# Four of the low parts of expert 1 made between the gathers of slots 7 and 8 instead of before all gathers

## The reference, cut to what matters

```python
x = attn_out.transpose(0, 2, 1, 3).reshape(B * S, H * D)
logits = xn @ en.T / tau                  # xn, en: rows of unit length
expert_idx = np.argmax(logits, axis=1)
gate_w = probs[np.arange(N), expert_idx]
for e in range(E):
    mask = expert_idx == e
    h = np.maximum(x[mask] @ w1[e], 0.0)
    out[mask] = gate_w[mask, None] * (h @ w2[e])
```

## Time and profile before

| what | value |
|---|---|
| median of 3 runs | 1118.97 us (1118.86 to 1122.63) |
| the profiled execution | 1119.63 us, of it the span 1118.0 us |
| mean granted TensorE clock | 0.977 |
| busy in the span | PE 94%, PEld 78%, DVE 57%, POOL 52%, ACT 45% |
| chain that ended last | PE 57%, POOL 6%, DMA 5% |

### The profile page before, as it was taken

The page is one execution under the profiler, slowest core; times in us unless marked ns, Lnnn a source line. Parts: engine busy times, 40 slices in busy tenths (PEclk is TensorE's granted clock), DMA queues, the critical chain, the costliest instruction groups (busy, mean ns, idle before and its releaser), DMA issues.

```text
span 1118.0 us, 21568 instructions
## 1 busy us (share of the span) xinstructions
PE 1050.3 (94%) x6536; PEld 873.2 (78%) x6536; DVE 631.7 (57%) x1477; ACT 508.5 (45%) x1035; POOL 579.8 (52%) x680
## 2 busy tenths in 40 slices
PE   7999999999993998999999995799999999999998
PEld 5777777777762887788888884698989999999997
DVE  6878878787856222121222212567767667676664
ACT  4666767666644222222222211355544545555543
POOL 3333333333334787877670602885656556565554
PEclk9999999999995999999999997899999999999999
DMA  4642414322345789989971814510101001010000
GB/s 118 177 116 80 112 55 118 89 78 80 99 156 158 245 255 266 300 282 308 301 244 54 268 49 130 180 29 2 57 1 57 1 6 52 0 56 0 29 1 29
DMA packets 102628, 129.62 MB, mean 116 GB/s; under 512 B 39520, under 2 KB 56928, under 8 KB 102048
## 3 DMA queue, kind: packets, MB, share of 16 engines
q1 hardware_dynamic: 78096, 68.38, 20.1%
q0 software_dynamic: 18880, 53.22, 15.5%
q10 hardware_dynamic: 5584, 7.16, 1.8%
HBM read 112.74 MB, written 15.99 MB: 115 GB/s over the span
## 4 chain that ended last, share of the span: by engine, by line
PE 57%; POOL 6%; DMA 5%; issue 2%; DVE 1%; ACT 1%; POOLq 0%; SPq 0%; DVEq 0%; ACTq 0%
PE ps L1032 17%; PE ps L1034 17%; PE ps L1033 17%; DMA stage<-w 3%; POOL wl L551 3%; PE ps L1058 1%; POOL woutl L551 1%; POOL wh L562 1%; PE ps L972 1%; PE ps L1028 1%; DMA wouth<-w_out 1%; PE ps L1107 1%; PE ps L982 1%; POOL xs_far L588 0%; ACT junk L773 0%
## 5 line engine op out<-in xcount | busy, mean ns | idle before, releaser
L551 POOL TENSOR_TENSOR wl<-stage,wh 128x512 fp32r<-128x512 f32 x128 | 161.9, 1290 | 60.6 <-DMA stage<-w 52.9
L663 POOL TENSOR_TENSOR mg<-mw,mr 128x384 f32<-128x384 f32 x96 | 118.6, 1235 | 75.4 <-DVE mr L1463 75.3
L711 ACT ACTIVATE ex<-sc,rmin 128x576 f32<-128x576 f32 x144 | 111.5, 775 | 94.7 <-DVE sc L1234 94.3
L1032 PE MATMUL ps<-yth,winh 128*128 128x384 f32 x384 | 132.6, 345 | 7.9 <-DVE mw L1451 7.9
L667 POOL TENSOR_TENSOR gl<-mg,gh 128x384 fp32r<-128x384 f32 x96 | 97.5, 1016 | 76.8 <-ACT gh L842 76.8
L1234 DVE TENSOR_SCALAR_CACHE_REDUCE sc<-ps,nscale 128x576 f32<-128x576 f32 x144 | 117.1, 814 | 28.6 <-PE ps L886 23.8
L1034 PE MATMUL ps<-yth,winl 128*128 128x384 f32 x384 | 130.6, 340 | 0.0
L1033 PE MATMUL ps<-ytl,winh 128*128 128x384 f32 x384 | 130.3, 339 | 0.0
L517 POOL TENSOR_SCALAR thr<-rmin,taup 128x1 f32<-128x1 f32 x144 | 66.2, 460 | 101.0 <-DVE sc L1234 100.0
L1034 PE MATMUL ps<-wouth,gl 128*128 128x512 f32 x288 | 114.2, 396 | 0.0
L1033 PE MATMUL ps<-woutl,gh 128*128 128x512 f32 x288 | 114.0, 396 | 0.0
(11 more groups left out here) (201 smaller groups left out, 2430.6 us busy)
## 6 DMA issues: line engine op xcount, KB each, us to landing
wh<-w POOLq DMA_DIRECT2D x32, 1024.0 KB, 9.1
stage<-w SPq DMA_DIRECT2D x128, 256.0 KB, 4.6
y_sorted<-yo ACTq DMA_DIRECT2D x25, 256.0 KB, 4.4
q_t<-qT SPq DMA_DIRECT2D x16, 288.0 KB, 2.8
k_t<-kT SPq DMA_DIRECT2D x16, 288.0 KB, 3.2
vb<-v SPq DMA_DIRECT2D x16, 288.0 KB, 3.4
out<-os SPq DMA_DIRECT2D x18, 256.0 KB, 3.1
stage<-w_in SPq DMA_DIRECT2D x16, 256.0 KB, 3.0
```

The costliest lines, as they stand in the source:

```text
L551: g.tensor_tensor(dst, raw, src.bitcast(F32), ALU.subtract).then_inc(w_split, 1)
L663: g.tensor_tensor(mg[:, f % 2, :], mw[:, f % 2, :], mr[:, f % 2, :], ALU.mult).then_inc(g_done, 1)
L711: act.activation(ex[:, i % 2, t * S:(t + 1) * S], sc[:, i % 2, t * S:(t + 1) * S], ACT.Exp, bias=rmin[:, i % 2, t:t + 1], scale=-1.0).then ...
L1032: pe.matmul(out_, lhs_h, rhs_h, start=start, stop=False)
```

## The change

Low quarter 1 of expert 1, four TENSOR_TENSOR on POOL with their waits, is moved from before the gathers to between gather 7 and gather 8 (2 * FIRST is 8).

```diff
         for i in range(QUARTERS):
             load_quarter(1, 1, i)
-        for i in range(2):
-            low_quarter(1, 1, 1, i)
+        low_quarter(1, 1, 1, 0)
...
         g.wait_ge(placed, 1)
-        for s in range(NEAR):
+        for s in range(2 * FIRST):
+            gather(s)
+        low_quarter(1, 1, 1, 1)
+        for s in range(2 * FIRST, NEAR):
             gather(s)
         g.wait_ge(gates_kept, 1)
```

## The result

| kernel | median | ratio to before, 95% interval |
|---|---|---|
| before | 1120.48 us (15 runs) | 1 |
| changed | 1125.01 us (15 runs, 1120.94 to 1127.34) | 1.0037 (1.0024 to 1.0049) |
| changed, measured again (e8) | 1122.59 us (12 runs) | 1.0026 (1.0013 to 1.0039) |
| changed, a third time (e11), on another chip | 1123.10 us (12 runs) | 1.0003 (0.9987 to 1.0018) |

A forecast was written before the change was run, and what follows sets the result against it. POOL's arrival at expert 2's loads was taken to bound the kernel: 2.5 us gained on DVE, 5.1 added on POOL, so 1118.97 + 2.6 = 1121.6 us, 0.23% slower; range 1118.2 to 1125.2.

The forecast's parts named there:

- The bound: Between the gathers and 475.6 us POOL sets the time; its arrival at expert 2's loads, 378.44, shifts all that follows.
- The gain on DVE: Before the gathers, three DVE operations freed from POOL's low parts bring the first gather 2.5 us earlier (2.35 to 2.66).
- the upper bound of 0.61: L1327 undisturbed on DVE takes at most 0.61 us, its end behind POOL's boundary; 0.45 was taken.
- the strict rule: A blocked DVE operation has its whole duration still ahead: L1327 needs 0.61 us, gain 2.35, sum 2.75; not adopted.
- The cost on POOL: Between gathers 7 and 8, four low parts add 5.1 us to POOL's way to expert 2's loads, nothing on DVE.
- the forecast sum: POOL reaches the loads of expert 2 at 378.44 - 2.5 + 5.1 = 381.04, 2.6 us later (2.4 to 2.8).
- it moves as a block: All in POOL's stretch from expert 2's loads to 475.5 us, issued by POOL or on its signals, shifts together by 2.6.
- slot 9 at 478.2, after a wait of about 1.5: PE starts slot 9 at 478.2 us in the profile after, released by POOL after waiting about 1.5 us.
- rival D: The longer gap puts slot 9's wait in a low clock or doubles the low time: at most 2.8 us, 1124.4; 0.05.
- Behind it nothing has changed its place relative to PE: After slot 9 starts, the rest of the kernel follows PE as before, so the end moves by the same 2.6 us.
- a longer wait at slot 7 costs no more: PE's slot 7 wait grows from 3.92 to about 9.0 us, with no larger low-clock loss than the 2.83 us before.

The follow-up runs named there:

- e8: The changed kernel again, no edit, on the chip of a later run; 1122.59 us, ratio 1.0026 to before.
- e11: The changed kernel a third time, no edit, on another chip; 1123.10 us, ratio 1.0003 to before.
- e1: The changed kernel with quarter 1's four low parts ahead of gather 0, behind the wait for placed, not between gathers 7 and 8; 1122.28 us, ratio 1.0020 to before.
- e4: The kernel before with quarter 1's low parts made on DVE in its idle time behind inv_i, none on POOL; 1119.30 us, ratio 0.9984 to before.
- e2: The kernel before, quarter 1 in its old place, plus four further subtractions on POOL between gathers 7 and 8; 1124.57 us, ratio 1.0030 to before.
- e3: The changed kernel with 30 transposes of the identity on PE ahead of m1 of slot 9; 1123.36 us, ratio 1.0022 to before.
- e5: As e4, with quarter 2 of expert 1 made on DVE too, behind its work for slot 0; 1113.49 us, ratio 0.9945 to before.
- e9: As e5, with quarter 3 of expert 1 made on DVE too, in its work for slot 1; 1114.39 us, ratio 0.9923 to before.
- e12: The kernel before, unchanged, measured against itself with a second profile; 1122.53 us, ratio 0.9990.

## Why the prediction was right, and where it was off

**The bound.** Right. e1 moved the start of slot 0 by 3.9 us at no cost. Counted from the first load of expert 1, POOL's arrival at the loads of expert 2 moved by -1.7 us in e4, +2.2 in e1, +2.6 in the changed kernel and in e8, and +3.9 in e2; the times moved, in the order of these kernels, by -1.8, +2.2, +4.1 and +2.9, and +3.4. All of these are on chips whose profiles show no holds; the +0.3 of e11 does not fit the row. "POOL's clock starts at 378.44, and whatever shifts that moment shifts all that follows" is what the runs show, to within about 1.5 us.

**The gain on DVE.** Forecast 2.5 us (2.35 to 2.66), measured 2.18 in the pair of profiles: 0.28 + 0.95 + 0.95. The term that was off is L1327. Alone it takes 0.77 us, above the upper bound of 0.61. The bound was read as the time from POOL's boundary to the operation's end. The two neighbours ended 0.15 and 0.17 us behind theirs while taking 0.31 alone, so some 0.15 us of an operation is already behind it when it is let go; 0.61 + 0.15 gives 0.76. The prediction had both numbers in hand and used them only against the strict rule. That the gain hangs on when the stage chunks land was missed altogether: it was 1.51 in e2. In the second profile of the kernel before the disturbed durations were 0.72, 0.31, 1.39 and 1.25, or 1.98 us above the undisturbed ones. The first gather still came at 349.48 against the forecast 349.6, since the attention ended 0.3 us earlier in that execution: that much of the agreement is luck.

The Trainium skill, "SBUF — State Buffer", section "Who interferes with whom", named the right pairs: of the operations beside POOL, those with two SBUF inputs were long, and the reduction at L1322, which lay wholly beside POOL, took 0.30 us before and after. That the later one is blocked for the whole of the other agrees with the ends: 0.15, 0.17 and 0.61 us behind POOL's boundaries. What the prediction called the strict reading, in which a blocked operation has all of its own duration still ahead of it, does not agree: those durations are 0.31, 0.31 and 0.77 us.

**The cost on POOL.** Forecast 5.1, measured 4.9: the next gather started 5.21 us behind gather 7's end, of which 0.30 stood there before. No DVE operation was slowed in the new place. The arrival at the loads, counted from the first load of expert 1, moved from 56.56 us (378.44 - 321.88) to 59.17 (380.73 - 321.56), by 2.6: the forecast sum. Gain and cost were each forecast 0.2 us too large, and cancel: from the first load to the first gather it is 2.3 us less, from there to the loads 4.9 more.

**The step that failed** is "it moves as a block", with "slot 9 at 478.2, after a wait of about 1.5". Slot 9 came 98.5 us behind POOL's arrival in place of 97.2, through other stage waits. POOL's waits from the loads to 480 us after:

```profile
POOL wl L551 <- DMA stage<-w: 22.4, 9, 5.8
```

The prediction had 20.8. PE had also reached slot 9 sooner, since slot 7 to slot 8 took 14.11 us against 15.08. The two add up to a wait of 4.15 us, and the clock fell: 1.6 us more. The event is that of rival D, given 0.05 and priced at up to 2.8. Its mechanism, that the longer gap at slot 7 brings it about, is not what the runs show: e4 with 5.00 us at slot 7 and e1 with 2.88 had waits at slot 9 of 3.56 and 4.39 us, and the clock fell in both. What they show is that the prediction took as fixed what scatters between executions: the stage waits (slot 9 stands 97.2 us behind the loads in one profile, 98.1 to 99.8 in seven others), the loss after slot 7 (2.8 us in one profile, 1.5 to 2.8 in the others), and the part behind the slots. "Behind it nothing has changed its place relative to PE" holds to about 2 us only, as the last slot shows. The prediction rightly said that a longer wait at slot 7 costs no more.

So the sum of 2.6 us is borne out on POOL and by e8 (+2.9 us). Why the first measurement gave +4.1 us stays open. Its mean granted clock of 0.9756 would fit more falls of the clock like that at slot 9, but e8, whose profile has the same fall, shows no lower mean clock than the kernel before.

## What to carry to other kernels

Idle time of an engine ahead of a stretch that it bounds is worth its full length: work placed in that idle time costs this engine nothing, and one position behind the signal that ends it, the same work costs all of its duration. Before work is moved out of another engine's way, weigh the interference (2 us here) against the work (5 us), and look for a third engine with idle time for it; here DVE, which does the same work in half the time. And a sum that is taken from one profiled execution carries the landing times of its DMAs: with terms of 2 us, a second profile of the old kernel is worth more than a second decimal. A difference of two spans that meets the forecast should be followed through the trace: here 5.2 us at slot 10 and 2.2 us back behind the slots made the 3.0 us.

## What was not expected of the hardware

- The length of a wait of PE alone did not decide whether the clock fell. Before slot 9, waits of 1.55, 2.17 (e3, behind the filler) and 2.38 us kept it. Waits at slots 7 and 9 from 2.59 us (e11, slot 7) to 9.54 us (e2, slot 7) all lost it. In the last slot a wait of 1.79 us lost it in the first profile of before and kept it in the one after. The loss did not grow with the wait: 2.83 us after 3.92, 1.9 after 8.85, 1.5 after 9.35 (e3), 2.8 after 9.54, 1.4 after 5.12 (e5).
- A TENSOR_TENSOR of 128x144 with its bf16 output written in another order than it is read took 0.77 us on DVE, against 0.30 for one of the same shape in order with f32 output. No run separates the order from the type; the prediction's row of 450 elements with bf16 output in order, 0.63 us, speaks for the order.
- A subtraction of 128x512 on POOL took 1.26 us with two different inputs and 1.01 us with the same tile as both.
- In e9 to e12, between 366 and 384 us, several engines had idle times of 2.3 to 7.9 us with "remote" as the releaser, which stands in none of the ten other profiles there, and PE gaps of 0.7 to 1.5 us with "issue" in three of them. What holds them is open.
